# In-chunk product with v as the stationary operand, on two column halves, and the loop re-ordered around it

## The chip, the cores and the metric

The kernel runs on one NeuronCore of a Trainium2 chip. The metric is the time of one execution in microseconds (us): 279.82 us, the median of three runs from 279.08 to 280.14 us. The engines are named as in the profile: PE is TensorE (matmuls; PEld its weight loads), DVE is VectorE, ACT is ScalarE, POOL is GpSimd, and SP is the engine that issues most transfers. SBUF is the working memory of 128 partitions. PSUM is the memory that PE writes to, in eight banks of 128 x 512 float32.

## The reference

The program computes three layers, one after another, on 2 batches of 768 tokens with 8 heads of 40 (width 320). The first is a gated recurrence. Its core, cut:

```
for t in range(S):
    m_new = np.maximum(f_gate[:, :, t] + m, i_gate[:, :, t])
    f_stab, i_stab = np.exp(f_gate[:, :, t] + m - m_new), np.exp(i_gate[:, :, t] - m_new)
    C = f_stab * C + i_stab * einsum('bhd,bhe->bhde', vt, kt)
    n = f_stab * n + i_stab * kt
    y[t] = sigmoid(o_gate[t]) * (C @ qt) / max(abs(n . qt), 1.0)
```

The second layer multiplies by `w_in` (320 x 1024) with a relu, splits the result into halves u and v, normalises v over its 512 columns, mixes v over the tokens with `w_spatial` (768 x 768), multiplies by u, and multiplies by `w_out` (512 x 320). The third multiplies by a second `w_in`, applies a convolution of three taps with a gate, and multiplies by a second `w_out`.

## The kernel before

The recurrence is computed in chunks of L = 128 tokens: NS = 12 chunks (6 for each batch), and a Python loop over the steps n = 1 to 11 writes the instructions of every engine out by hand. Nothing is scheduled by a program: each engine works through its own list in order and waits on semaphores. A step holds one chunk of the recurrence, and beside it pieces of the second layer for earlier chunks. In step n PE does, in this order:

- `scores(n)` (L506): k times q for 8 heads, 8 matmuls with 40 rows each, for even and odd heads in two row halves of the array.
- `transpose_x(n - 1)` (L542): three transposes of x, the finished output of the recurrence for chunk n-1.
- `from_state(n)` (L514): q times the state that chunk n-1 left. It is left out at n = 6, the first chunk of the second batch.
- `in_chunk(n, 0)` (L536): scores times decay is the stationary operand (128 x 128), and `v_aug` (v with two more columns for the denominator, 42 columns for a head) the moving one: 4 matmuls for 4 heads. The result `intra` is 128 tokens by 8 x 42.
- `hidden_v(n - 1)` (L559): 8 matmuls of x with the v half of `w_in`, 512 columns wide.
- `in_chunk(n, 1)`, and `to_state(n + 1)` (L525): k times v for the next state.
- `hidden_u` (L578): 16 matmuls of x of two chunks with the u half.

A float32 matmul appears as two rows in the profile, a transpose and a float32r matmul as one.

DVE multiplies the scores by the decay (`weigh`, L983), splits x (`xt_low`, L1084 and L1086), weighs what comes from the state (`weigh_inter`, L1058), makes the new state (`new_state`, L1051), takes mean and variance of an earlier chunk's hidden v (`moments`, L1091), writes the low part of its normalised v (`vn_low(n - 3)`, L1104) and of a piece of `w_spatial` (`spatial_low`, L1179, from step 6 on), and then combines: numerator (L1065 or L1067), denominator (L1069), reciprocal (L1071), their product (L1073), and x by the output gate (L1079).

ACT splits x as well (`xt_high`, L758 and L759), normalises v of chunk n-3 into z (L774) and copies z to float32r (`vn_high`, L781), applies the relu of u (L768), computes the decay matrices of the next chunk with 8 exponentials of 128 x 128 (`exp_log`, L751, two groups of four), and the relu of v (`v_relus`, L786). In steps 5 to 10 it also rounds a piece of `w_spatial` (`spatial_high`, L791). POOL masks the logarithms, weighs k, decays the state and takes the power for the deviation (L387).

After the loop come 16 `spatial` products (L592) with the rest of layer two between them, and then layer three (L634 and L649).

Of the kernel before, what the change touches and what calls it, by code (L numbers as in the profile page):

```python
# [9 lines left out]
L = 128  # L10
NC = S // L
NS = B * NC
G = 2
# [42 lines left out]
def build_program(nc, qk, k, v, ig, fg, og, w_in, w_sp, b_sp, w_out, w_in2, conv, w_out2, neg_m, out):  # L56
    sems = {}

    def sem(name):
        if name not in sems:  # L60
# [28 lines left out]
             for i, at in enumerate((vn_at, vnlo_at))]  # L89
    o_gate = lambda n: og_b0[:, n, :] if n < NC else og_b1[(n - NC) // 3][:, n % 3, :]  # L90
# [102 lines left out]
    intra = banks[3][:, 0:H * DV].rearrange("p (h d) -> p h d", h=H)  # L193
# [6 lines left out]
    p_cols = banks[4].rearrange("p (i r) -> p i r", i=4)  # L200
    p_mix, p_x = banks[0:2], banks[2:8]
# [6 lines left out]
    by_head = lambda i, n: cols[:, i, n * H:(n + 1) * H].rearrange("p (g j) -> p j g", g=G)  # L208
    pairs = lambda t: t.rearrange("p (j g) d -> p j g d", g=G)
    spatial_step = lambda c: 5 + c  # L210
# [6 lines left out]
    heads = lambda t: t.rearrange("p (h d) -> p h d", h=H)  # L217
# [24 lines left out]
    def sync_program(sp):  # L242
# [22 lines left out]
        def load_v(n):  # L265
            if n >= RING:
                sp.wait_ge(sem("intra_ready"), 2 * (n - RING + 1))
            sp.dma_start(v_aug[n % RING][:, :, :].rearrange("p h d -> p (h d)"), v[n, :, :]
                         ).then_inc(sem(f"ld_v{n % RING}"), 16)
# [17 lines left out]
        load_qk(0)  # L287
        load_in(v_half, "v")
        load_v(0)
# [17 lines left out]
        for n in range(1, NS):  # L307
            if gives_state(n) and ki(n) + KRING < B * (NC - 1):
                load_k(state_chunk(ki(n) + KRING))
            if n + RING < NS:  # L310
                load_qk(n + RING)
                load_log(n + RING)
                load_v(n + RING)
# [25 lines left out]
    def gpsimd_program(pool):  # L339
# [62 lines left out]
        narrow_low(0, v_half)  # L402
        pool.wait_ge(sem("cols_ready"), 4)
        weigh_k(0)
        mask_first(1, 0)
        mask_first(1, 1)
        mask_log(2)
        weigh_k(1)
        decay_state(1)
        weigh_k(2)  # L410
        decay_state(2)
        for n in range(2, NS):
            if n == 2:
                pool.wait_ge(sem("x_ready"), 2)
            if n + 1 < NS:
                mask_log(n + 1)
            if n == 2:
                narrow_low(1, u_half)
            if gives_state(n + 1):
                weigh_k(n + 1)  # L420
                if has_state(n + 1):
                    decay_state(n + 1)
            if n > spatial_step(0):
                spatial_low(n - 1 - spatial_step(0))
            if n > 1:
                deviation(n - 2)
# [23 lines left out]
    def tensor_program(pe):  # L450
        def keep_warm(times):
            for _ in range(times):
                pe.matmul(p_warm[:, 0:2 * L], xt_hi[0][:, 0, 0:128], xt_hi[0][:, 0, :], start=True, stop=True)
# [213 lines left out]
        for n in range(1, NS):  # L667
            scores(n)
            if n == 2:
                from_state(n)  # L670
            transpose_x(n - 1)
            if has_state(n) and n != 2:
                from_state(n)
            in_chunk(n, 0)
            hidden_v(n - 1)
            if n == 1:
                to_state(n)
            in_chunk(n, 1)
            if gives_state(n + 1):
                to_state(n + 1)  # L680
            if n > 1:
                hidden_u(group(n - 2), n % 2)
# [31 lines left out]
    def scalar_program(act):  # L714
# [39 lines left out]
        def xt_high(n):  # L754
# [4 lines left out]
            act.activation(xt5[p][0:K5, cs], p_t[0:K5, 2 * L:3 * L], ACT.Copy).then_inc(sem("xt_hi_ready"), 1)  # L759

# [99 lines left out]
        def narrow_copy(half, cs):  # L860
# [8 lines left out]
        act.activation(win5_lo[LO:128, :].rearrange("p (x t) -> p x t", x=8),  # L869
                       ident[LO:128, :].unsqueeze(1).to_broadcast([LO, 8, 128]), ACT.Copy, scale=0.0).then_inc(sem("win_ready"), 1)  # L870
        narrow_high("v", v_half)
        win_high("v", v_half)
        pad_log(0)
        exp_log(1, 0)
        narrow_copy("v", v_half)
        for n in range(1, NS):
            if n == LATE + 1:
                xt_high(n - 1)
            exp_log(n, 1)
            if n == 1:  # L880
                xt_high(0)
            if n == 2:
                win_high("u", u_half)
                narrow_high("u", u_half)
                xt_high(1)
                narrow_copy("u", u_half)
# [3 lines left out]
            if n not in (1, 2, LATE + 1):  # L890
                xt_high(n - 1)
            if n == 2:
                open_gates(1)
            if n > 2:
                normalise(n - 3)
                vn_high(n - 3)
                ut_relu(group(n - 3), (n - 3) % 2)
# [3 lines left out]
            if n + 1 < NS:  # L901
                exp_log(n + 1, 0)
            if n == 1:
                pad_log(1)
            v_relus(n - 1)
        normalise(NS - 3)
        vn_high(NS - 3)
        ut_relu(group(NS - 3), 1)
# [424 lines left out]
```

## Time and profile before

| | |
|---|---|
| median of 3 runs | 279.82 us (279.08 to 280.14) |
| profiled execution, its own time | 278.94 us |
| its span | 277.1 us, so 1.8 us lie around it |
| PE busy | 269.2 us (97%) |
| DVE, ACT, POOL busy | 202.4 (73%), 165.7 (60%), 69.0 us (25%) |
| granted PE clock | 1.00 (2.4 GHz) in every stretch of the loop |
| chain that ended last | PE 83%, DVE 7%, ACT 6%, issue 2%, DMA 1% |

The span has three parts: a start up to step 1 (0 to 15.4 us), the loop (to 108.7 us), and the stages behind it. Busy time of PE counts a matmul to its modelled end, and neighbours overlap; the distance between the starts of two blocks is what a block takes from PE.

### The profile page before, as it was taken

Reading aid. Unit: us, or ns where it says so; the run is one execution under the profiler, and the core shown is the slowest. Engines: PE = TensorE matmul, PEld = TensorE weight load, DVE = VectorE, ACT = ScalarE, POOL = GpSimd, SP = SyncE. Lnnn points to the kernel's source line nnn. Section 1 sums busy time; section 2 is a strip of 40 time slices with the busy share of each in tenths; the row PEclk is TensorE's granted clock in tenths of the full one; section 3 lists DMA queues with packets and bytes.
Section 4 is the critical chain, followed back from the end, with each engine's and each line's share of the span. In section 5 each row is a group of like instructions: output and inputs, shape, how many; then the busy total and the mean of one; then the engine's idle time right before and its main releaser. Section 6 shows DMA issues by size and latency. Waiting matters only on the chain.

```text
span 277.1 us, 5247 instructions
## 1 busy us (share of the span) xinstructions
PE 269.2 (97%) x1959; PEld 257.6 (93%) x1959; DVE 202.4 (73%) x367; ACT 165.7 (60%) x329; POOL 69.0 (25%) x101
## 2 busy tenths in 40 slices
PE   8889999999999999999999999999999999999995
PEld 6777989889999999999999999999999999999995
DVE  5687987787988988655467686456867776876694
ACT  7968877996886664323243212256576567666763
POOL 6484532166454322063000790000000000000000
PEclk9999999999999999999999999999999999999999
DMA  6789975465546000009400000000000000300004
GB/s 176 227 229 285 296 231 196 143 207 160 184 117 228 2 0 2 0 0 269 151 0 2 0 0 2 0 0 0 4 0 2 0 0 2 142 0 4 0 0 146
DMA packets 13258, 23.61 MB, mean 85 GB/s; under 512 B 1968, under 2 KB 7920, under 8 KB 13232
## 3 DMA queue, kind: packets, MB, share of 16 engines
q1 hardware_dynamic: 12832, 22.89, 27.1%
q8 instruction: 16, 0.26, 0.4%
q10 hardware_dynamic: 400, 0.38, 0.4%
q14 instruction: 10, 0.08, 0.1%
HBM read 21.25 MB, written 2.02 MB: 84 GB/s over the span
## 4 chain that ended last, share of the span: by engine, by line
PE 83%; DVE 7%; ACT 6%; issue 2%; DMA 1%; SPq 0%; DVEq 0%; ACTq 0%
PE bank L592 18%; PE bank L649 14%; PE bank L634 14%; PE bank L617 8%; PE bank L578 7%; PE bank L559 7%; PE bank L536 6%; PE bank L506 3%; PE bank L514 2%; PE bank L542 1%; DMA og_b<-og 1%; PE bank L525 1%; DVE win_lo L988 1%; ACT decay L751 1%; DVE decay L983 1%
## 5 line engine op out<-in xcount | busy, mean ns | idle before, releaser
L592 PE MATMUL bank<-wsp_hi,vn_hi 128*128 128x384 f32 x96 | 32.2, 335 | 0.0
L592 PE MATMUL bank<-wsp_lo,vn_hi 128*128 128x384 f32 x96 | 32.1, 334 | 0.0
L592 PE MATMUL bank<-wsp_hi,vn_lo 128*128 128x384 f32 x96 | 32.1, 334 | 0.0
L796 ACT ACTIVATE gt_hi<-gated_t 128x384 fp32r<-128x384 f32 x16 | 8.4, 524 | 37.1 <-DVE gated_t L1117 37.1
L649 PE MATMUL bank<-wo_hi,hg_hi 128*128 128x320 f32 x96 | 29.8, 311 | 0.3 <-DVE hg_lo L1167 0.3
L649 PE MATMUL bank<-wo_lo,hg_hi 128*128 128x320 f32 x96 | 29.6, 308 | 0.0
L649 PE MATMUL bank<-wo_hi,hg_lo 128*128 128x320 f32 x96 | 29.6, 308 | 0.0
L1150 DVE SCALAR_TENSOR_TENSOR tap<-h,conv_w,tap 128x768 f32<-128x768 f32 (+1 forms) x17 | 16.5, 970 | 17.5 <-ACT tap L828 17.5
L751 ACT ACTIVATE decay<-log_in,cols 128x128 f32<-128x128 f32 x80 | 25.5, 391 | 4.1 <-PE bank L536 4.0
L536 PEld LDWEIGHTS bank<-v_aug,decay 128*128 128x128 f32 x192 | 24.0, 191 | 2.6 <-DVE decay L983 1.3
L834 ACT ACTIVATE gate<-convd 128x768 f32<-128x768 f32 (+1 forms) x17 | 13.8, 809 | 19.3 <-DVE convd L1154 19.3
L536 PE MATMUL bank<-v_aug,decay 128*128 128x42 f32 x192 | 24.3, 278 | 1.0 <-DVE decay L983 0.6
L387 POOL TENSOR_TENSOR rstd<-var_eps,minus_half 128x1 f32<-128x1 f32 x12 | 9.7, 805 | 50.8 <-DVE var_eps L1095 50.8
L634 PE MATMUL bank<-x_hi,win_hi 128*128 128x384 f32 x64 | 21.4, 335 | 0.0
L634 PE MATMUL bank<-x_lo,win_hi 128*128 128x384 f32 x64 | 21.4, 335 | 0.0
L634 PE MATMUL bank<-x_hi,win_lo 128*128 128x384 f32 x64 | 21.4, 335 | 0.0
L983 DVE TENSOR_TENSOR decay<-bank,decay 128x512 f32<-128x512 f32 x24 | 16.5, 687 | 4.7 <-PE bank L506 3.2
L817 ACT ACTIVATE h<-bank 128x384 f32<-128x384 f32 x32 | 15.3, 486 | 7.2 <-PE bank L634 7.2
L1113 DVE TENSOR_TENSOR mixed<-bank,bias_sp 128x384 f32<-128x384 f32 x16 | 8.9, 554 | 13.6 <-PE bank L592 13.6
L649 PEld LDWEIGHTS bank<-wo_hi,hg_hi 128*128 128x128 f32 x96 | 18.0, 187 | 0.7 <-issue 0.6
L1161 DVE TENSOR_TENSOR hg<-h,gate 128x768 f32<-128x768 f32 (+1 forms) x17 | 15.5, 910 | 3.7 <-ACT gate L834 3.7
L592 PEld LDWEIGHTS bank<-wsp_lo,vn_hi 128*128 128x128 f32 x96 | 18.0, 188 | 0.0
(171 smaller groups left out, 766.7 us busy)
## 6 DMA issues: line engine op xcount, KB each, us to landing
qk<-qk SPq DMA_DIRECT2D x24, 160.0 KB
log_in<-neg_m SPq DMA_DIRECT2D x10, 256.0 KB, 5.0
wsp_raw<-w_sp SPq DMA_DIRECT2D x6, 384.0 KB, 3.9
win_raw<-w_in SPq DMA_DIRECT2D x4, 512.0 KB, 5.6
v_aug<-v SPq DMA_DIRECT2D x12, 168.0 KB, 4.4
kw<-k SPq DMA_DIRECT2D x10, 160.0 KB, 4.9
out<-y SPq DMA_DIRECT2D x10, 160.0 KB, 1.9
og_b<-og SPq DMA_DIRECT2D x3, 480.0 KB, 9.9
```

The lines of the kernel that those rows point to most:

```text
L536: op = pe.matmul(intra[:, h, :], decay[g][:, j * L:(j + 1) * L], v_aug[n % RING][:, h, :], start=True, stop=True)
L559: op = pe.matmul(p_v[:, :], lhs, rhs, start=(i == 0), stop=(i == len(products) - 1))
L578: op = pe.matmul(p_u[:, d * 2 * L:(d + 1) * 2 * L], lhs, rhs, start=(i == 0), stop=(i == len(products) - 1))
L592: op = pe.matmul(p_mix[m % 2][:, 0:NB], vs[:, b * NC + c, ds_], ws[:, c, ts], start=(i == 0), stop=(i == len(terms) - 1))
L617: op = pe.matmul(p_x[i % 6][:, 0:NB], w, gs, start=(k_ == 0), stop=(k_ == len(products) - 1))
L634: op = pe.matmul(p_h[blk][:, 0:NB], w, xx, start=(i == 0), stop=(i == len(terms) - 1))
L649: op = pe.matmul(p_y[c][:, 0:HD], g[t % 2][:, cs], w[:, t, :], start=(t == 0 and i == 0), stop=(t == KF - 1 and i == 2))
L751: op = act.activation(dst, src, ACT.Exp, bias=cols[:, 2, r:r + 1], scale=1.0 if n else -1.0)
L817: act.activation(h2[t % 2][:, 1 + blk * NB:1 + (blk + 1) * NB], p_h[blk][:, 0:NB], ACT.Relu).then_inc(sem("relu_done"), 1)
L983: dve.tensor_tensor(decay[g][:, :], p_s[g][:, :, :].rearrange("p h t -> p (h t)"), decay[g][:, :], ALU.mult).then_inc(sem("weights_ready"), 1)
L1150: dve.scalar_tensor_tensor(tap01[:, cs], h2[t % 2][:, moved(cs, 1)], cw[:, t, 1:2], tap0[:, cs], ALU.mult, ALU.add).then_inc(sem("tap01_do ...
L1161: dve.tensor_tensor(hg[e % 2][:, cs], h2[e % 2][:, moved(cs, 1)], gate2[e % 2][:, cs], ALU.mult).then_inc(sem("hg_done"), 1)
```

## The change

The product inside a chunk swaps its operands. `v_aug` of one head (128 x 42) is now the stationary operand, and the decayed scores (128 x 128) move. The result is transposed: 42 rows (numerator and denominators) by 128 tokens. Heads with even j go to columns 0 to 41 of the array and PSUM partitions 0 to 41, heads with odd j to columns and partitions 64 to 105. Keys and v of `to_state` had such halves already. ACT copies the result (106 x 512) from PSUM to SBUF (`num_t`), and PE turns it back with four transposes into a bank that from step 2 on is the first bank of the scores. DVE reads it there. Its combining is split into `numerators(n)` (numerator, denominator, reciprocal) and `combine(n)` (the division in its own step, then the gate). `scores(n)` therefore waits for `numer_done`, and `in_chunk` for `numer_moved`.

The lists of all engines are re-ordered, the load of v stands earlier on SP, and v's ring waits for `to_state` too. A memset moves from ACT to DVE. The diff, cut:

```
-    intra = banks[3][:, 0:H * DV].rearrange("p (h d) -> p h d", h=H)
+    intra_t = banks[3].rearrange("p (g x t) -> p g x t", g=G, x=2)
+    turned_bank = lambda n: p_t if n == 0 else p_u if n == 1 else banks[1]
...
         def scores(n):
+            if n > 2:
+                pe.wait_ge(sem("numer_done"), n)
...
         def in_chunk(n, g):
-                wait(pe, sem("numer_done"), n)
+            if n:
+                pe.wait_ge(sem("numer_moved"), n)
             for j in range(HG):
-                h = head(g, j)
-                op = pe.matmul(intra[:, h, :], decay[g][:, j * L:(j + 1) * L], v_aug[n % RING][:, h, :], start=True, stop=True)
+                x_, c = divmod(j, 2)
+                op = pe.matmul(intra_t[c * LO:c * LO + DV, g, x_, :], v_aug[n % RING][:, head(g, j), :],
+                               decay[g][:, j * L:(j + 1) * L], start=True, stop=True)
+        def turn_back(n):
+            pe.wait_ge(sem("numer_moved"), n + 1)
+            for g in range(G):
+                for x_ in range(2):
+                    at = (2 * g + x_) * 128
+                    op = pe.transpose(turned_bank(n)[:, at:at + LO + DV], num_t[:, g, x_, :], ident[0:LO + DV, 0:LO + DV])
+            op.then_inc(sem("numer_turned"), 1)
...
+        for n in range(2, NS):
+            if n > 2:
+                scores(n)
+            transpose_x(n - 1)
+            if has_state(n):
+                from_state(n)
+            elif gives_state(n):
+                to_state(n)
             in_chunk(n, 0)
+            in_chunk(n, 1)
+            if has_state(n) and gives_state(n):
+                to_state(n)
             hidden_v(n - 1)
+            turn_back(n)
+            hidden_u(group(n - 2), n % 2)
...
+        def move_numer(n):
+            act.wait_ge(sem("intra_ready"), 2 * n + 2)
+            wait(act, sem("numer_turned"), n)
+            act.activation(num_t[:, :, :, :], intra_t[0:LO + DV, :, :, :], ACT.Copy).then_inc(sem("numer_moved"), 1)
...
+        for n in range(3, NS):
+            xt_high(n - 1)
+            normalise(n - 3)
+            move_numer(n)
+            if n + 1 < NS:
+                exp_log(n + 1, 0)
+                exp_log(n + 1, 1)
+            v_relus(n - 1)
+            vn_high(n - 3)
...
+        for n in range(2, NS):
             if n > 2:
                 minus_mean(n - 3)
             weigh(n, 0)
+            weigh(n, 1)
             xt_low(n - 1)
             if has_state(n):
                 weigh_inter(n)
+            if gives_state(n):
                 new_state(n)
...
+            moments(n - 2)
             if n > 2:
                 vn_low(n - 3)
             if n > spatial_step(0):
                 spatial_low(n - 1 - spatial_step(0))
+            numerators(n)
+            combine(n)
```

ACT in step 7 of the loop, before (a name with a number behind it is one buffer of a ring; the brackets hold the semaphores waited for):

```order
L758 ACTIVATE xt_hi_90<-bank 128x2x128 [waits ut_raw,xt_raw]
L759 ACTIVATE xt_94<-bank 64x128
L774 ACTIVATE z<-v_relu_95,shift,rstd 128x512 [waits vn_ready,shift_ready]
L781 ACTIVATE vn_hi<-z 128x512 [waits z_ready]
L768 ACTIVATE uT<-bank 128x2x256 [waits ut_raw]
L751 ACTIVATE decay_81<-log_in_100,cols 128x128 [waits intra_ready,log_masked]
L751 ACTIVATE decay_81<-log_in_100,cols 128x128 x3
L786 ACTIVATE v_relu_95<-bank 128x512 [waits z_ready,vh_ready]
L751 ACTIVATE decay_82<-log_in_100,cols 128x128 [waits intra_ready,log_masked]
L751 ACTIVATE decay_82<-log_in_100,cols 128x128 x3
L791 ACTIVATE wsp_hi<-wsp_raw 128x384 [waits ld_wsp3] x2
```

and ACT in the same step now:

```order
L783 ACTIVATE xt_hi_91<-bank 128x2x128 [waits ut_raw,xt_raw]
L784 ACTIVATE xt_95<-bank 64x128
L804 ACTIVATE z<-v_relu_96,shift,rstd 128x512 [waits vn_ready,shift_ready]
L789 ACTIVATE num_t<-bank 106x512 [waits numer_turned,intra_ready]
L776 ACTIVATE decay_82<-log_in_101,cols 128x128 [waits intra_ready,log_masked]
L776 ACTIVATE decay_82<-log_in_101,cols 128x128 x3
L776 ACTIVATE decay_83<-log_in_101,cols 128x128 [waits intra_ready,log_masked]
L776 ACTIVATE decay_83<-log_in_101,cols 128x128 x3
L816 ACTIVATE v_relu_96<-bank 128x512 [waits z_ready,vh_ready]
L811 ACTIVATE vn_hi<-z 128x512 [waits z_ready]
L821 ACTIVATE wsp_hi<-wsp_raw 128x384 [waits ld_wsp2] x2
```

The copy of z to `vn_hi` stood directly behind z. Now the new copy `num_t`, all eight exponentials and the relu of v stand ahead of it.

DVE in the second part of step 7, before:

```order
L1091 BN_STATS stats<-v_relu_95 128x6 [waits v_relu_ready]
L1093 BN_AGGR mv<-stats 128x2 [waits mom1]
L1095 TENSOR_SCALAR var_eps<-mv 128x1 [waits mom2]
L1104 TENSOR_TENSOR vn_lo<-z,vn_hi 128x512 [waits vn_hi_ready]
L1179 TENSOR_TENSOR wsp_lo<-wsp_raw,wsp_hi 128x384 [waits wsp_hi]
L1065 TENSOR_TENSOR numer<-bank,mix 128x336 [waits mix_done,intra_ready]
L1069 SCALAR_TENSOR_TENSOR denom<-numer 128x8 [waits numer_done]
```

and now:

```order
L1128 BN_STATS stats<-v_relu_96 128x6 [waits v_relu_ready]
L1130 BN_AGGR mv<-stats 128x2 [waits mom1]
L1132 TENSOR_SCALAR var_eps<-mv 128x1 [waits mom2]
L1141 TENSOR_TENSOR vn_lo<-z,vn_hi 128x512 [waits vn_hi_ready]
L1216 TENSOR_TENSOR wsp_lo<-wsp_raw,wsp_hi 128x384 [waits wsp_hi]
L1100 TENSOR_TENSOR numer<-bank,mix 128x336 [waits mix_done,numer_turned]
L1104 SCALAR_TENSOR_TENSOR denom<-numer 128x8 [waits numer_done]
```

The order of these rows is the same. The numerator waits for the turned result instead of the product itself.

PE around the product in step 7, before (the first of the eight instructions of `hidden_v` alone):

```order
L514 MATMUL bank<-state_86,qk_73 128x84 [waits mix_done,state_done]
L514 MATMUL bank<-state_86,qk_73 128x84 x3
L536 MATMUL bank<-v_aug_79,decay_81 128x42 [waits numer_done,ld_v1,weights_ready]
L536 MATMUL bank<-v_aug_79,decay_81 128x42 x3
L559 MATMUL bank<-win_hi,xt_hi_90 128x512 [waits v_relu_ready,xt_ready]
```

and now, from `scores` on:

```order
L512 MATMUL bank<-qk_74 128x128 [waits numer_done,weights_ready,ld_qk1]
L512 MATMUL bank<-qk_74 128x128 x7
L558 MATMUL bank<-ident,x 128x128 [waits x_ready]
L558 MATMUL bank<-ident,x 128x128
L558 MATMUL bank<-ident,x 64x128
L520 MATMUL bank<-state_87,qk_74 128x84 [waits mix_done,state_done]
L520 MATMUL bank<-state_87,qk_74 128x84 x3
L543 MATMUL bank<-decay_82,v_aug_80 42x128 [waits numer_moved,ld_v1,weights_ready]
L543 MATMUL bank<-decay_82,v_aug_80 42x128 x3
L543 MATMUL bank<-decay_83,v_aug_80 42x128 [waits numer_moved,weights_ready]
L543 MATMUL bank<-decay_83,v_aug_80 42x128 x3
L531 MATMUL bank<-v_aug_80,kw_76 40x42 [waits ld_v1,state_done,kw_ready]
```

Both halves of the product stand side by side, `to_state` behind them, and `scores` has the wait for `numer_done` that `in_chunk` had.

## Rows read from the trace of the kernel before

**Rows 1.** The chain that ended last, in order of time: start us, us, what

```profile
10.22 1.05 ACT win_lo L869
...
12.91 1.46 DVE win_lo L988
...
48.83 1.28 ACT L751
...
75.59 1.09 PE bank L506 x16
...
78.02 0.86 PE bank L536 x8
78.88 1.92 PE bank L559 x8
80.80 0.82 PE bank L536 x8
...
82.05 2.11 PE bank L578 x16
84.16 1.09 PE bank L506 x16
...
108.74 3.13 PE bank L592 x18
```

**Rows 2.** Step 7: us, busy PE, PEld, DVE, ACT, POOL, clock, DMA share, GB/s

```profile
66.95:75.52 8.57, 8.57 (x84) 7.87 (x83) 7.37 (x18) 6.24 (x16) 4.47 (x5) 1.00 0.55 175
```

**Rows 3.** PE in order of time: start us, us, engine, instruction

```profile
10.17 1.08 PE L483 MATMUL bank<-gate_padded,ident 128*128 128x128 f32 x8
...
33.63 0.55 PE L542 MATMUL bank<-ident,x 128*128 128x128 f32 x3
...
68.05 0.55 PE L542 MATMUL bank<-ident,x 128*128 128x128 f32 x3
68.43 1.02 PE L514 MATMUL bank<-state,qk 104*128 104x84 f32 x8
69.29 1.02 PE L536 MATMUL bank<-v_aug,decay 128*128 128x42 f32 x8
72.98 0.51 PE L525 MATMUL bank<-v_aug,kw 128*40 128x42 f32 x16
```

**Rows 4.** ACT in step 7, in order of time

```profile
69.91 0.63 ACT L781 ACTIVATE vn_hi<-z 128x512 fp32r<-128x512 f32 x1
70.44 0.58 ACT L768 ACTIVATE uT<-bank 128x512 f32<-128x512 f32 x1
70.92 1.27 ACT L751 ACTIVATE decay<-log_in,cols 128x128 f32<-128x128 f32 x4
72.27 0.60 ACT L786 ACTIVATE v_relu<-bank 128x512 f32<-128x512 f32 x1
```

**Rows 5.** DVE in steps 7 and 11, in order of time

```profile
71.98 0.68 DVE L1104 TENSOR_TENSOR vn_lo<-z,vn_hi 128x512 fp32r<-128x512 f32 x1
72.58 0.55 DVE L1179 TENSOR_TENSOR wsp_lo<-wsp_raw,wsp_hi 128x384 fp32r<-128x384 f32 x1
73.09 0.51 DVE L1065 TENSOR_TENSOR numer<-bank,mix 128x336 f32<-128x336 f32 x1
73.63 0.58 DVE L1069 SCALAR_TENSOR_TENSOR denom<-numer 128x8 f32<-128x8 f32 x1
74.25 0.20 DVE L1071 RECIPROCAL rdenom<-denom 128x8 f32<-128x8 f32 x1
74.48 0.77 DVE L1073 TENSOR_TENSOR numer<-numer,rdenom 128x320 f32<-128x320 f32 x1
75.29 0.49 DVE L1079 TENSOR_TENSOR x<-numer,og_b 128x320 f32<-128x320 f32 x1
...
107.33 0.17 DVE L1069 SCALAR_TENSOR_TENSOR denom<-numer 128x8 f32<-128x8 f32 x1
107.78 0.49 DVE L1073 TENSOR_TENSOR numer<-numer,rdenom 128x320 f32<-128x320 f32 x1
```

More of the change, by code:

```diff
@@ L418, in gpsimd_program @@
                 narrow_low(1, u_half)
+            if n > spatial_step(0):
+                spatial_low(n - 1 - spatial_step(0))
             if gives_state(n + 1):
@@ L422, in gpsimd_program @@
                     decay_state(n + 1)
[L423 to L426, printed above, removed]
+            deviation(n - 2)
         deviation(NS - 2)
@@ L451, in keep_warm @@
         def keep_warm(times):
-            for _ in range(times):
-                pe.matmul(p_warm[:, 0:2 * L], xt_hi[0][:, 0, 0:128], xt_hi[0][:, 0, :], start=True, stop=True)
+            for i in range(times):
+                half = slice((i % 2) * 2 * L, (i % 2 + 1) * 2 * L)
+                pe.matmul(p_warm[:, half], xt_hi[0][:, 0, 0:128], xt_hi[0][:, 0, :], start=True, stop=True)
         pe.wait_ge(sem("warm_zero"), 1)
@@ L666, in tensor_program @@
         to_state(0)
-        for n in range(1, NS):
-            scores(n)
-            if n == 2:
+        turn_back(0)
+        scores(1)
+        from_state(1)
+        in_chunk(1, 0)
+        in_chunk(1, 1)
+        to_state(1)
+        transpose_x(0)
+        turn_back(1)
+        scores(2)
+        hidden_v(0)
+        for n in range(2, NS):
[3 more added lines that the diff above has]
+            if has_state(n):
                 from_state(n)
-            transpose_x(n - 1)
-            if has_state(n) and n != 2:
-                from_state(n)
+            elif gives_state(n):
+                to_state(n)
             in_chunk(n, 0)
+            in_chunk(n, 1)
+            if has_state(n) and gives_state(n):
+                to_state(n)
             hidden_v(n - 1)
[L676 to L682, printed above, removed]
+            turn_back(n)
+            hidden_u(group(n - 2), n % 2)
         spatial(0)
@@ L868, in scalar_program @@
         exp_log(0, 1)
-        act.activation(win5_lo[LO:128, :].rearrange("p (x t) -> p x t", x=8),
-                       ident[LO:128, :].unsqueeze(1).to_broadcast([LO, 8, 128]), ACT.Copy, scale=0.0).then_inc(sem("win_ready"), 1)
         narrow_high("v", v_half)
         win_high("v", v_half)
+        exp_log(1, 0)
+        move_numer(0)
+        exp_log(1, 1)
         pad_log(0)
-        exp_log(1, 0)
         narrow_copy("v", v_half)
[L876 to L886, printed above, removed]
+        pad_log(1)
+        move_numer(1)
+        xt_high(0)
+        exp_log(2, 0)
+        exp_log(2, 1)
+        v_relus(0)
+        win_high("u", u_half)
+        xt_high(1)
+        narrow_high("u", u_half)
+        move_numer(2)
+        narrow_copy("u", u_half)
+        exp_log(3, 0)
+        exp_log(3, 1)
+        v_relus(1)
+        open_gates(1)
+        ut_relu(0, 0)
+        for n in range(3, NS):
[7 more added lines that the diff above has]
+            vn_high(n - 3)
             if spatial_step(0) <= n < spatial_step(NC):
@@ L1182, in vector_program @@
         first_low(0, v_half)
-        for n in range(1, NS):
-            combine(n - 1)
-            if n == 1:
-                new_state(0)
+        new_state(0)
+        numerators(0)
+        weigh(1, 0)
+        weigh(1, 1)
+        combine(0)
+        weigh_inter(1)
+        new_state(1)
+        xt_low(0)
+        numerators(1)
+        combine(1)
+        for n in range(2, NS):
             if n > 2:
                 minus_mean(n - 3)
-            if gives_state(n) and n > 2:
-                new_state(n)
             weigh(n, 0)
-            if n == 2:
-                new_state(n)
+            weigh(n, 1)
             xt_low(n - 1)
@@ L1196, in vector_program @@
                 weigh_inter(n)
-            weigh(n, 1)
-            if n == 1:
+            if gives_state(n):
                 new_state(n)
```

59 lines of the change are left out of this document (25 added, 34 removed).

## The prediction

> **What bounds the kernel now.** I read the chain that ended last first: PE carries 83% of it, and from 60 us on the loop is nothing but PE blocks in a row. One step, from `scores` to `scores`, is 84.16 - 75.59 = 8.57 us [rows 1]. The table by stretches says the same of step 7: PE is busy for 8.57 of 8.57 us, DVE for 7.37, ACT for 6.24, and the granted clock is 1.00 [rows 2]. So a step is PE's work, ACT has 2.3 us of air, and DVE 1.2. Then I read each engine in order of time through step 7 [rows 3 to 5], because the change re-orders all lists, and asked of every wait how late its releaser would now be. That, and not the busy shares, decides here.
>
> **What PE saves.** The product takes 0.86 + 0.82 us in a step, 16 instructions of 0.107 us [rows 1]. These have 42 moving columns, and `from_state` takes the same 0.86 us to the next start with 84 [rows 3]: what is paid is the 128-column stationary operand. New: 16 instructions with 42 stationary and 128 moving columns, alternating between two column halves. The trace does not show this form. Its nearest row for moving columns is `scores`: 16 instructions with 128 moving columns on two row halves, 1.09 us with the switch, or 1.16 us to the modelled end [rows 1, 3]. Less its share of switching I take 0.93 us (16 x 0.058, that is 1.16 less a tail of about 0.25, over 16). The upper end is no overlap: 8 instructions of 128 moving on 128 stationary columns take 1.08 us, a little more than the 1.02 us of the old product [rows 3], so 0.11 us each, 1.76 us for 16. The lower end is `to_state`, 16 in column halves in 0.51 us [rows 3], but with a third of the columns. Four transposes come on top: three of x take 0.38 us to the next start [rows 3], so 0.5 us for four. PE then needs 8.57 - 1.68 + 0.93 + 0.5 = 8.32 us, 0.25 less a step. If PE remained the bound, eleven steps would give about 2.8 us.
>
> **The wait that the order creates.** ACT used to write `vn_hi` right behind z, 69.91 us in step 7, when PE was just in the first half of the product [rows 3, 4]. Now the new copy of the result, all eight exponentials and the relu of v stand ahead of it. DVE's list has `vn_low(n - 3)`, which reads `vn_hi`, and `spatial_low` ahead of `numerators(n)`. Behind the numerator hang two things: `scores(n + 1)`, whose bank it frees, and, through denominator, ratio and gate, x for `transpose_x(n)`, which is queued ahead of `from_state` and the product of the next step. The copy on ACT in turn waits for that product. So this is a closed ring through PE, ACT and DVE, and it must be run once a step, however fast PE is.
>
> The Trainium skill bears on it. The page "TensorEngine Tiling (Array Packing)", section "Performance Considerations", says that tiling speeds up TensorE but not the evacuation of PSUM, which may become the bottleneck. It would have the faster product lose what the copy out of PSUM costs. It gives no time here; rows 4 and 5 price it.
>
> **The ring, from transpose to transpose.** PE: hand-over 0.04, transposes to the next start 0.38, `from_state` 0.86, product to its end 1.16 (as `scores`) [rows 3]. Hand-over 0.04. ACT: the copy of 512 columns out of PSUM like that of u, 0.58 us, but the next starts after 0.48; twice four exponentials 2.40 (4 in 1.27, less the overlap of neighbours); relu 0.50; `vn_hi` 0.63 to its end [rows 4]. Hand-over 0.04. DVE: `vn_lo` 0.60, `wsp_lo` 0.51, numerator 0.54 start to start. That is 8.18 us. Denominator 0.21 to 0.62, reciprocal 0.23, ratio 0.53 to 0.81, x 0.49 [rows 5]: the low values are those of step 11, the high ones of step 7, where POOL worked at the same time. Sum 9.64 to 10.33 us. By the other edge, `scores(n + 1)` can end at 8.18 + 0.04 + 1.09 = 9.3 us, so x is later. PE alone would be back at 8.32. The ring wins by 1.3 to 2.0 us, and PE stands idle for them. Before step 6 there is no `spatial_low` on DVE, and the ring is 9.13 to 9.82.
>
> The relu of v does not stretch it: `hidden_v` ends 0.38 + 0.86 + 0.93 + 0.44 + 1.92, with a tail about 4.8 us after the transposes' start, and ACT is through its exponentials only at 5.4. DVE's own work in front (two `weigh`, `xt_low`, `mix`, new state, moments) is done by about 6 us, `vn_hi` comes at 6.5. What ACT has behind `vn_hi` (rounding of `w_spatial`, relu of u) is hidden in the wait of the next step for its transposes.
>
> **The sum.** Eight rings lie between the transposes of steps 3 and 11: three without and five with `spatial_low`, 3 x 9.13 + 5 x 9.64 = 75.6 at the low, 3 x 9.82 + 5 x 10.33 = 81.1 at the high end. After each opening of output gates ACT loads its exponential table, 1.28 us [rows 1]; this now stands in the ring in steps 3 and 5: + 2.56. Step 6 has no `from_state` but `to_state` ahead of the product: - 0.86 + 0.44. From the transposes of step 11 PE is the bound again, its list has no `to_state` and no exponentials follow: 0.38 + 0.86 + 0.93 + 1.92 + 0.5 + 2.11 = 6.7. Together 84.4 to 89.9 us, against 108.74 - 33.63 = 75.1 us before [rows 1, 3]: 9.3 to 14.8 more.
>
> The start, up to the transposes of step 3, I expect to be shorter. Before, the chain went through a memset of 1.05 us on ACT and the split of `w_in` of 1.46 us on DVE, one after another, ahead of the first numerator [rows 1]. The memset goes to DVE, which waits for PE at that time, and the split now runs beside the first copy and turn. Against these 2.5 us stand the copies and turns of chunks 0 and 1, 0.5 us each, of which about half should show. I take 1.6 us less, between 0 and 3. The earlier load of v and its ring's longer wait cost nothing: loads run three chunks ahead. Behind the loop nothing changes: x of chunk 11 is due only after the first `spatial` product of 3.13 us [rows 1].
>
> Sum: middle 12.1 - 1.6 = 10.5 us longer. The profiled execution took 278.94 us, so it gives 289.4; it lies 0.9 below the median of the runs, 279.82 us, and on that scale I predict 290.3 us.
>
> **Rivals.**
> *The halves do not overlap.* Then the product in the ring takes 0.83 us more (1.76 against 0.93), eight times: 6.6 us, 297 us. For it speaks that all 128 rows are in use by both halves, which is not so in `scores`. Against it: 16 instructions of `to_state` in column halves take 0.51 us to their end [rows 3], about 0.03 each, which leaves hardly any room for loads and matmuls of two halves one after another. The Trainium skill, "TensorE: Matmul & The Clock Gate", section on packing small matmuls, states that weight loads overlap running matmuls only where the row group differs; that would give this rival's 297 us. The same page reports a speed-up for column packing, and no row here shows the weight load of 42 beside 128 moving columns.
> *PE remains the bound, faster.* If `vn_hi` were written early enough, each step would be PE's 8.32 us. The point from which it decides: `vn_hi` must be there before 5.3 us after the transposes' start, so that the numerator is ready at PE's return at 7.2; by the rows it comes at 6.5. It would need two fewer groups of exponentials ahead of it. Price: 2.8 us from the steps and 1.6 from the start, 275.4 us. For it: PE is the bound in all of rows 1. Against it: the lists as they stand.
> *The ring is there, but shorter.* If neighbours on ACT and DVE overlap more and POOL never disturbs DVE, 9.0 us a ring with a start that gains 3 us: about 284 us.
> *The ring grows,* with POOL's halves of `spatial_low` now beside DVE's: 0.5 us more in five rings, 293 us. I hold this in the forecast's own range, 286 to 294.5.
>
> **How the numbers follow.** Forecast 0.76 (290.3 us), no overlap 0.10 (297), shorter ring 0.08 (284), PE the bound 0.05 (275.4), the rest, about the same time, 0.01. The range, 285 to 296, leaves out most of the first and last rivals. One measurement of this kernel tells 0.5% (1.4 us) from no change: faster 0.05, same 0.02, slower 0.93.
>
> **What would show it.** In the profile after: PE idle ahead of the transposes of x, released by DVE x, for 1 to 2 us a step, or ahead of `scores` released by the numerator; DVE idle ahead of `vn_lo`, released by ACT `vn_hi`; transposes of x 9.6 to 10.3 us apart in steps 7 to 11; the product's 16 instructions in 1.2 us; the first `spatial` product at 117 to 121 us instead of 108.7, and the stretch behind it as long as before. DVE never waiting for `vn_hi` would prove the ring wrong. The product in 1.9 us would show the halves one after another. An end of the start later than 33.6 us would put my 1.6 us on the wrong side.

## The result, and the profile after

| | before | after |
|---|---|---|
| median of four runs (least, most), us | 279.45 (278.83, 280.14) | 309.13 (307.52, 311.44) |
| profiled execution, its span, us | 278.94, 277.1 | 307.52, 305.8 |
| transposes of x of step 3 start, us | 33.63 | 36.60 |
| first `spatial` product starts, us | 108.74 | 137.11 |
| from there to the end of the span, us | 168.4 | 168.7 |

The ratio is 1.1068, with the interval [1.0986, 1.1149]. A median is over all runs of a kernel, while a ratio and its interval leave out the runs more than 1.5% above the kernel's fastest; without these the medians of e1 and e6 below are 280.92 and 278.32 us. I had predicted 290.3 us in a range of 285 to 296: the sign was right, the size far off. By the profiled executions the span grew by 28.7 us where I had 10.5. The miss of 18.2 lies in two places. The start came 3.0 us later instead of 1.6 earlier (4.6). From the transposes of step 3 to the first `spatial` product it took 100.5 us, where my sum gave 84.4 to 89.9, middle 87.15 (13.4). The rest is 0.3, behind the loop.

The page of the kernel after: busy times, the granted clock in 40 slices, the chain by engine.

```profile
PE 278.8 (91%) x2007; PEld 262.4 (86%) x2007; DVE 207.8 (68%) x368; ACT 169.9 (56%) x340; POOL 66.4 (22%) x101
...
PEclk9998995997776879999999999999999999999999
...
PE 67%; DVE 13%; ACT 12%; issue 5%; DMA 2%; SPq 0%; ACTq 0%; DVEq 0%
```

PE had 83% of the chain before; DVE and ACT now have 25% together. The clock row is the one I had not foreseen: it held 9 in all 40 slices before, and now has eight below that among the first 15. The waits of after (us in total, times, longest):

```profile
DVE vn_lo L1141 <- ACT vn_hi L811: 22.3, 9, 4.4
...
PE bank L512 <- DVE numer L1100: 12.8, 7, 2.4
...
PE bank L558 <- DVE x L1116: 4.7, 7, 2.3
```

These are the three joints of the ring that I predicted, in its order: ACT to DVE, DVE to `scores`, DVE to the transposes. The chain of waits through step 10, which answers to the step of [rows 1]:

```profile
119.76 0.55 PE bank L558 x3
120.30 0.86 PE bank L520 x8
121.16 1.03 PE bank L543 x16
...
122.71 2.45 ACT decay L776 x8
125.16 0.48 ACT v_relu L816
125.64 0.53 ACT vn_hi L811
...
126.80 1.35 DVE wsp_lo L1216
...
128.19 0.52 DVE numer L1100
```

The next transposes start at 130.25, a step of 10.49 us. Compare term by term with my low sum of 9.64. From the transposes to the end of the product PE takes 2.43 us, where I had 2.40; copy, exponentials, relu and numerator stand as written. The new product's 16 instructions take 1.03 us of the chain. One term is off: `wsp_lo` is 1.35 us, where [rows 5] have 0.55. The difference, 0.8, is nearly the whole of 10.49 - 9.64.

Step 10 was the only late step at full clock. Stretches of after: three around step 4, then step 7 beside step 10 (us, busy PE, PEld, DVE, ACT, POOL, clock, DMA share, GB/s); they answer to [rows 2].

```profile
44.00:46.00 2.00, 0.15 (x2) 0.18 (x4) 1.43 (x4) 0.92 (x2) 0.00 (x0) 1.00 0.41 151
46.00:48.00 2.00, 2.00 (x19) 1.74 (x19) 1.59 (x5) 0.00 (x0) 0.00 (x0) 0.59 0.26 83
48.00:50.00 2.00, 2.00 (x12) 1.85 (x12) 1.61 (x4) 1.25 (x3) 0.00 (x0) 0.50 0.00 0
...
82.36:94.84 12.48, 10.71 (x88) 9.51 (x87) 8.08 (x18) 6.63 (x17) 4.51 (x5) 0.77 0.40 118
119.76:130.25 10.49, 8.22 (x88) 7.33 (x88) 7.95 (x20) 6.50 (x17) 1.64 (x2) 1.00 0.00 0
```

PE is busy 0.15 of 2 us, and when it has work again the clock is 0.59, then 0.50: the lower of its two levels, 1.2 GHz. Steps 7 and 10 have the same 88 instructions; at 0.77 they keep PE busy for 10.71 us, at 1.00 for 8.22. What that looks like in order of time, where step 6 ends and step 7 begins (it answers to [rows 3 to 5]):

```profile
77.75 0.69 DVE L1141 TENSOR_TENSOR vn_lo<-z,vn_hi 128x512 fp32r<-128x512 f32 x1 [3.29 <-ACT vn_hi L811]
...
78.21 1.09 POOL L398 TENSOR_TENSOR wsp_lo<-wsp_raw,wsp_hi 128x384 fp32r<-128x384 f32 x1 [2.01 <-ACT wsp_hi L821]
78.35 1.35 DVE L1216 TENSOR_TENSOR wsp_lo<-wsp_raw,wsp_hi 128x384 fp32r<-128x384 f32 x1
...
80.39 2.03 PE L512 MATMUL bank<-qk 40*128 40x128 f32 x16 [2.35 <-DVE numer L1102]
...
82.36 0.90 PE L558 MATMUL bank<-ident,x 128*128 128x128 f32 x3
...
83.05 1.84 PE L520 MATMUL bank<-state,qk 104*128 104x84 f32 x8
...
84.82 1.94 PE L543 MATMUL bank<-decay,v_aug 128*42 128x128 f32 x16
```

Three things stand here at once. DVE waited 3.29 us for `vn_hi`: the ring. DVE's `wsp_lo` and POOL's overlap, and DVE's ends 0.4 us behind POOL's: 1.35 us. PE then stood idle for 2.35 us, and `scores`, transposes, `from_state` and product take 2.03, 0.90, 1.84 and 1.94 us, where [rows 1, 3] have 1.09, 0.55 and 1.02 and step 10 has 1.08 for the product. All four lie in the ring: x was there at 81.74, but at this clock `scores`, which is queued ahead of the transposes, ends only at 82.42, so even the edge that I had as the shorter one (9.3 against 9.64) decides.

The start, in order of time:

```profile
10.91 0.63 ACT L888 ACTIVATE win_hi<-win_raw 64x512 fp32r<-64x512 f32 x1 [0.85 <-DMA win_raw<-w_in]
...
12.53 1.48 DVE L1019 TENSOR_TENSOR win_lo<-win_raw,win_hi 128x1024 fp32r<-128x1024 f32 x1 [0.42 <-ACT win_hi L884]
...
14.74 0.51 DVE L1102 COPY numer<-bank 128x336 f32<-128x336 f32 x1
...
17.00 0.74 POOL L375 TENSOR_TENSOR state_dec<-state,dec 104x336 f32<-104x336 f32 x1
17.09 2.81 DVE L1110 TENSOR_TENSOR numer<-numer,rdenom 128x320 f32<-128x320 f32 x1
17.70 1.14 POOL L387 TENSOR_SCALAR_AFFINE_SELECT log_in<-log_in 128x1024 f32<-128x1024 f32 x1
18.82 0.73 POOL L370 TENSOR_TENSOR kw<-kw,cols 128x320 f32<-128x320 f32 x1
...
20.48 0.55 PE L558 MATMUL bank<-ident,x 128*128 128x128 f32 x3 [2.31 <-DVE x L1116]
...
30.02 2.47 DVE L1019 TENSOR_TENSOR win_lo<-win_raw,win_hi 128x1024 fp32r<-128x1024 f32 x1
```

The ratio takes 0.49 us when nothing is beside it [rows 5]; here 2.81, until POOL's three instructions in a row are over, and PE waits 2.31 us. The split of `w_in`'s second half, 2.47 us, stands ahead of the numerator of chunk 2. It stood there before as well, and took 1.77 us:

```profile
28.14 1.77 DVE L988 TENSOR_TENSOR win_lo<-win_raw,win_hi 128x1024 fp32r<-128x1024 f32 x1
```

The clock fell in the start too, behind PE's wait of 2.31 us. It was 1.00 in this time before. The stretch from there, then the eight instructions of `hidden_v(0)` in the chain:

```profile
20.48:24.00 3.52, 3.52 (x27) 2.98 (x28) 3.11 (x10) 2.91 (x10) 0.75 (x1) 0.78 1.07 253
```

```profile
22.49 3.63 PE bank L575 x8
```

In the run e2 below, which has the same instructions up to step 3, the ratio took as long (2.79 us) and PE waited 2.29 us for x, but the clock stayed at 1.00, `hidden_v(0)` took 2.08 us of the chain, and the transposes of step 3 came at 35.03 us instead of 36.60.

### The profile page after: what moved, and what is told of

Its sections match the earlier page's. It is cut to its first block, busy times and chain, and to the rows that moved or that the text cites. A ratio compares the mean times of both kernels' runs of the same rounds, so it can differ in the third digit from the quotient of the medians.

```text
span 305.8 us, 5384 instructions
## 1 busy us (share of the span) xinstructions
PE 278.8 (91%) x2007; PEld 262.4 (86%) x2007; DVE 207.8 (68%) x368; ACT 169.9 (56%) x340; POOL 66.4 (22%) x101
## 4 chain that ended last, share of the span: by engine, by line
PE 67%; DVE 13%; ACT 12%; issue 5%; DMA 2%; SPq 0%; ACTq 0%; DVEq 0%
PE bank L608 16%; PE bank L665 13%; PE bank L650 13%; PE bank L633 7%; ACT decay L776 5%; PE bank L543 4%; PE bank L575 3%; PE bank L520 3%; PE bank L558 2%; DVE wsp_lo L1216 2%; DVE numer L1110 2%; PE bank L512 2%; DMA win_raw<-w_in 2%; ACT vn_hi L811 2%; DVE numer L1100 1%
## 5 line engine op out<-in xcount | busy, mean ns | idle before, releaser
L512 PE MATMUL bank<-qk 40*128 40x128 f32 (+1 forms) x192 | 15.6, 306 | 15.7 <-DVE numer L1100 12.8
L512 PEld LDWEIGHTS bank<-qk 40*128 40x128 f32 (+1 forms) x192 | 13.3, 205 | 17.6 <-issue 16.5
L776 ACT ACTIVATE decay<-log_in,cols 128x128 f32<-128x128 f32 x80 | 24.6, 394 | 0.1
L1141 DVE TENSOR_TENSOR vn_lo<-z,vn_hi 128x512 fp32r<-128x512 f32 x12 | 8.9, 738 | 22.3 <-ACT vn_hi L811 22.3
L783 ACT ACTIVATE xt_hi<-bank 128x256 fp32r<-128x256 f32 x12 | 4.6, 384 | 28.7 <-PE bank L558 28.7
L608 PEld LDWEIGHTS bank<-wsp_hi,vn_hi 128*128 128x128 f32 x96 | 18.0, 188 | 0.3 <-DVE wsp_lo L1216 0.3
L608 PEld LDWEIGHTS bank<-wsp_hi,vn_lo 128*128 128x128 f32 x96 | 18.0, 188 | 0.0
```

The costliest lines, as they stand in the source:

```text
L512: op = pe.matmul(p_s[g][:, j, :], qk_n[ps, 1, j, :], qk_n[ps, 0, j, :], start=True, stop=True)
L608: op = pe.matmul(p_mix[m % 2][:, 0:NB], vs[:, b * NC + c, ds_], ws[:, c, ts], start=(i == 0), stop=(i == len(terms) - 1))
L776: op = act.activation(dst, src, ACT.Exp, bias=cols[:, 2, r:r + 1], scale=1.0 if n else -1.0)
```

## The experiments

The ratios are to the kernel before. Unless said otherwise an edit is made on the kernel after. "Steps" are the times between the transposes of x of two steps, "the loop" is from those of step 3 to the first `spatial` product: 75.1 us before, 100.5 after.

| run | median us | ratio | clock of the profiled execution |
|---|---|---|---|
| e1_vn_early | 282.45 | 1.0074 [1.0041, 1.0108] | 0.992 |
| e2_numer_first | 286.10 | 1.0243 [1.0211, 1.0275] | 0.994 |
| e3_keep_warm | 298.68 | 1.0681 [1.0621, 1.0742] | 0.994 |
| e4_pool_late | 310.90 | 1.1111 [1.1043, 1.1178] | 0.927 |
| e5_warm_quiet_ring | 292.99 | 1.0500 [1.0440, 1.0561] | 0.988 |
| e6_vn_quiet | 279.87 | 0.9964 [0.9922, 1.0005] | 0.987 |
| e7_vn_start | 277.08 | 0.9914 [0.9879, 0.9950] | 0.998 |
| e8_all | 274.51 | 0.9816 [0.9781, 0.9852] | 1.000 |
| e9_same_half | 283.40 | 1.0142 [1.0088, 1.0196] | 1.000 |
| e10_old_ring | 312.41 | 1.1239 [1.1165, 1.1314] | 0.928 |

### Is it the ring? Cut it at either joint

**e1**, ACT writes `vn_hi` ahead of the copy and the exponentials:

```diff
             normalise(n - 3)
+            vn_high(n - 3)
             move_numer(n)
...
             v_relus(n - 1)
-            vn_high(n - 3)
```

> The changed kernel with one edit: ACT copies z to vn_hi right behind z, ahead of the new copy and the exponentials. Theory 1 (the ring through ACT's list makes PE wait, and the idle time lets the clock fall): the ring opens, each step is PE's 8.3 us, the clock stays at 1.00 from step 4 on, eight steps and the tail take about 73 us instead of 100.5: 280 to 284 us. Rival (the new form of the product with its two copies makes PE slow or lets the clock fall by itself): the clock stays near 0.95 over the span and the time over 295 us.

One line moved takes 26.7 us off the medians, nearly all that the change cost. Steps 3 to 10 are 7.90 to 9.08 us and the loop 74.3. DVE's `vn_lo` waits for nothing now, and the clock is 1.00 in every stretch of 10 us from 40 to 110. What is left over is DVE's tail in steps 7 to 9. In order of time:

```profile
76.42 1.00 POOL L398 TENSOR_TENSOR wsp_lo<-wsp_raw,wsp_hi 128x384 fp32r<-128x384 f32 x1
...
76.75 1.03 DVE L1110 TENSOR_TENSOR numer<-numer,rdenom 128x320 f32<-128x320 f32 x1
...
77.81 0.91 DVE L1116 TENSOR_TENSOR x<-numer,og_b 128x320 f32<-128x320 f32 x1
...
78.77 0.44 PE L558 MATMUL bank<-ident,x 128*128 128x128 f32 x2 [0.89 <-DVE x L1116]
```

Ratio and gate take twice their 0.49 beside POOL, and PE waits 0.89 us for x.

**e2**, the other joint: DVE's numerator goes ahead of the two instructions that wait for ACT:

```diff
             moments(n - 2)
+            numerators(n)
+            combine(n)
             if n > 2:
                 vn_low(n - 3)
             if n > spatial_step(0):
                 spatial_low(n - 1 - spatial_step(0))
-            numerators(n)
-            combine(n)
```

> The changed kernel with one edit on DVE alone: numerators and combine ahead of vn_low and spatial_low, so the ring is cut at its other joint and ACT is left as it is. Theory 1: the numerator is ready at PE's return, 8.3 to 8.6 us a step, 281 to 286 us, though vn_hi is as late as ever. Rival (ACT is simply too full with the copy): DVE waits elsewhere for ACT, over 295 us.

It also ends the ring: 23.0 us less than after, with ACT's order as it was. A cost that sat in ACT's list alone, or in the product, would have stayed. It is slower than e1: in its step 7, which took 10.86 us, the numerator waited 1.19 us for the turned product, the gate ran beside POOL for 1.18 us, and the clock fell to 0.84.

**e10**, the same list made in the kernel *before*, with its old product: `vn_hi` behind both groups of exponentials.

```diff
             if n == LATE + 1:
+                vn_high(n - 4)
                 xt_high(n - 1)
             exp_log(n, 1)
+            if n > 3 and n != LATE + 1:
+                vn_high(n - 4)
...
                 normalise(n - 3)
-                vn_high(n - 3)
...
+        vn_high(NS - 4)
```

> The kernel before, with its own product and its own lists, and one edit: ACT copies z to vn_hi only behind the exponentials of both groups (for steps 0 to 8). Theory 1 (the order of the lists costs the time, not the new product): the same ring arises, by the rows of before 0.38 + 0.86 + 0.86 + 1.92 + 0.82 + 0.25 on PE, 1.2 + 0.63 on ACT, and about 3.1 on DVE: 10.1 us a step instead of 8.57, 291 to 296 us, more where the clock falls in the idle time. Rival (only the new product with its copy has such a ring): 279 to 281 us.

The kernel without any of the change becomes as slow as the one with it, 1.1239. It was expected at 291 to 296 us, more where the clock falls, and lies 16 us above that. In order of time:

```profile
80.71 1.85 PE L536 MATMUL bank<-v_aug,decay 128*128 128x42 f32 x8
...
89.10 0.69 DVE L1107 TENSOR_TENSOR vn_lo<-z,vn_hi 128x512 fp32r<-128x512 f32 x1 [6.04 <-ACT vn_hi L781]
...
92.23 0.55 PE L542 MATMUL bank<-ident,x 128*128 128x128 f32 x3 [1.43 <-DVE x L1082]
```

The step up to there took 13.26 us, at a clock of 0.74; how much of it is the ring and how much the clock was not run apart. So the place of `vn_hi` is enough for the loss, and the form of the product is not needed for it.

### What does the clock cost?

**e3** fills PE's idle time ahead of `scores` with nine matmuls (two instructions each in the trace) of the identity into columns of a bank that nothing reads then:

```diff
+            if n > 3:
+                pe.wait_ge(sem("state_done"), ki(n - 1) + gives_state(n - 1))
+                for _ in range(9):
+                    pe.matmul(banks[0][:, 384:512], ident[:, :], ident[:, :], start=True, stop=True)
```

> The changed kernel with 9 extra float32 matmuls of 128 x 128 into unused columns of a bank, ahead of scores from step 4 on, where PE stands idle for about 2.3 us; the result does not use them. The ring stays. Theory 1: the clock stays at 1.00 and steps 6 to 10 take 10.1 to 10.5 us instead of 12 to 12.8: about 10 us less, 297 to 301 us. Rival (the long steps come from the ring alone, the clock is a reading): 308 to 310 us.

PE does 144 instructions more, and the kernel is 10.45 us faster than after by the medians. The clock is 1.00 in every stretch of 10 us from 40 to 110. One step, by stretch:

```profile
101.88:112.36 10.48, 10.22 (x105) 9.34 (x106) 7.95 (x20) 6.48 (x17) 3.51 (x4) 1.00 0.01 2
```

Steps 6 to 10 are 9.98, 10.48, 10.49, 10.48 and 10.48 us: step 10 of after in every step (step 6, without `from_state`, is shorter as forecast). The loop takes 90.5 us against 100.5, so 10.0 us of the loss in the loop is the clock. In step 4 the extra matmuls themselves stand in the chain, for 2.01 us, so the clock cost is at least this. The busy share no longer tells where the bound is here: PE is busy for 10.22 of 10.48 us, in part with work that means nothing.

### What does POOL cost?

**e4** puts POOL's half of `spatial_low` back behind its scaling of the state, as it was before:

```diff
-            if n > spatial_step(0):
-                spatial_low(n - 1 - spatial_step(0))
             if gives_state(n + 1):
                 weigh_k(n + 1)
                 if has_state(n + 1):
                     decay_state(n + 1)
+            if n > spatial_step(0):
+                spatial_low(n - 1 - spatial_step(0))
```

> The changed kernel with POOL's half of spatial_low put back behind the decay of the state, as it was before the change, so that it no longer runs beside DVE's half. If the two halves together cost DVE 0.84 us in each of five steps (1.35 or 1.39 us against 0.51 us, inside the ring): 4 to 5 us less, 304 to 305 us, perhaps more where the shorter idle time keeps the clock up. Rival (DVE's half is slow because of something else): 309 us.

No gain, where 304 to 305 us were expected; the interval covers the ratio of after. Steps 7 to 10 take 12.70 to 13.13 us, none of them at full clock. The reason in order of time:

```profile
87.37 1.16 POOL L387 TENSOR_SCALAR_AFFINE_SELECT log_in<-log_in 128x1024 f32<-128x1024 f32 x1
87.84 1.94 DVE L1141 TENSOR_TENSOR vn_lo<-z,vn_hi 128x512 fp32r<-128x512 f32 x1 [1.60 <-ACT vn_hi L811]
88.49 0.74 POOL L370 TENSOR_TENSOR kw<-kw,cols 128x320 f32<-128x320 f32 x1
...
89.70 0.55 DVE L1216 TENSOR_TENSOR wsp_lo<-wsp_raw,wsp_hi 128x384 fp32r<-128x384 f32 x1
```

`wsp_lo` is at its 0.55, but now `vn_lo` stands beside the mask and the keys and takes 1.94 instead of 0.69. The collision had moved, not gone.

**e5** takes away all of it: e4's move, a wait that starts POOL's row only after x, and three filling matmuls for the clock:

```diff
+            if n > 2:
+                pool.wait_ge(sem("x_ready"), n)
             if n + 1 < NS:
                 mask_log(n + 1)
```

> The ring as in the changed kernel, with both things that lengthen it taken away: 3 extra matmuls in PE's idle time ahead of scores hold the clock, and POOL waits for x at the head of a step, so that its masks, keys and its half of spatial_low are done before DVE comes to vn_lo. If the ring was right in its terms and only these two were missed, steps 6 to 10 take the predicted 9.64 us (6: 9.2), steps 3 and 4 9.2 to 10.5, and the time is 290 to 293 us. Rival (POOL is not what stretches DVE's operations): steps of 10.5 us and 297 to 299 us.

Here is the bare ring, in order of time:

```profile
93.45 0.69 DVE L1147 TENSOR_TENSOR vn_lo<-z,vn_hi 128x512 fp32r<-128x512 f32 x1 [1.86 <-ACT vn_hi L817]
94.06 0.55 DVE L1222 TENSOR_TENSOR wsp_lo<-wsp_raw,wsp_hi 128x384 fp32r<-128x384 f32 x1
94.64 0.51 DVE L1106 TENSOR_TENSOR numer<-bank,mix 128x336 f32<-128x336 f32 x1
...
95.62 0.49 DVE L1116 TENSOR_TENSOR numer<-numer,rdenom 128x320 f32<-128x320 f32 x1
96.15 0.49 DVE L1122 TENSOR_TENSOR x<-numer,og_b 128x320 f32<-128x320 f32 x1
```

Steps 7 to 10 are 9.68, 9.67, 9.69 and 9.67 us, and my low sum was 9.64; step 6 is 9.18 against 9.22. Against e3 this is 0.8 us a step. Before step 6 three matmuls did not hold the clock (0.79 in 40 to 50 us, 0.87 in 50 to 60), and steps 3 to 5 took 10.63, 11.86 and 10.51 us instead of the expected 9.2 to 10.5, so e5's total is not a clean sum of the parts.

### Can the ring be cut and the rest mended?

**e6** is e1 with e5's two edits on POOL, without filling matmuls; its diff is those two.

> vn_hi early, and POOL waits for x as in the run above. With vn_hi early alone steps 7 and 8 took 9.0 us, since ratio and x on DVE were stretched to 1.03 and 0.91 us beside POOL. Theory (the two engines exclude each other): 8.35 us in all steps, ratio and x 0.49 each, 2 to 3 us less than with vn_hi early alone: 278 to 279 us. Rival (PE's own work): no change, 281 us.

The loop takes 72.0 us, 2.3 less than e1, with steps of about 8.34, PE's own. The medians differ by 2.6 us. In the profiled execution (281.37 us, in the upper part of 276.50 to 282.57) the transposes of step 3 are at 39.06 us: the start took back what the loop gave. One instruction of DVE there, the denominator of chunk 0, lasts 3.78 us, and the clock was 0.68 in 20 to 30 us.

**e7** is e1 with four edits in the start: ACT's two copies of `w_in`'s u half ahead of the relu of v, DVE's split of it ahead of the split of x (`xt_low`), the numerator of chunk 0 taken apart so that its inverse comes behind `weigh(1, 0)` and `weigh(1, 1)`, and POOL's first row behind x:

```diff
         weigh_k(1)
         decay_state(1)
+        pool.wait_ge(sem("x_ready"), 1)
         mask_log(2)
...
-        numerators(0)
+        numer_only(0)
         weigh(1, 0)
         weigh(1, 1)
+        inverse(0)
```

> vn_hi early, and the start changed: POOL waits for x of chunk 0 ahead of the mask of chunk 2, the denominators of chunk 0 stand behind the weights of chunk 1, and w_in's u half is rounded and split ahead of the relu of v and of xt_low(1). Theory (the start is late because a DVE operation of 0.5 us waited 2.8 to 3.6 us for a row of POOL operations, and because the split of 2.47 us stands ahead of the numerator of chunk 2): the transposes of step 3 come at 33 to 34 us instead of 37.0, 3 us less, 278 us. Rival (the start waits for PE and transfers): under 1 us.

Transposes of step 3 at 32.55 us, 4.5 before e1's 37.04; the clock is 1.00 in every stretch of the start, where e1 had 0.86 in 20 to 30 us; the loop is e1's, 74.2. The four were not run apart, so how much each gives is open.

**e8** has all of it: e6 and e7 together.

> vn_hi early, POOL quiet and the start changed together. Theory: both gains add, 275 to 277 us, below the kernel before (279). Rival: what one edit saves, the other had saved already, 278 us.

Faster than both kernels: 0.9816 of before, 34.6 us less than after. The loop takes 72.0 us and begins at 31.86. A step by stretch:

```profile
72.47:80.81 8.34, 8.15 (x87) 7.29 (x87) 7.67 (x20) 6.68 (x17) 4.53 (x5) 1.00 0.67 228
```

This is the gain that I had worked out for PE: 8.32 us a step against 8.57. It is small beside what a late `vn_hi` costs.

### Does the product need its two halves side by side?

**e9** is e1 with the four heads in the order 0, 2, 1, 3, so that two neighbours fall into the same column half:

```diff
-            for j in range(HG):
+            for j in (0, 2, 1, 3):
```

> vn_hi early, and within each group of four heads the order of the product is 0, 2, 1, 3: four instructions on one column half and then four on the other, instead of two and two. If the two halves run at the same time, the 16 instructions take longer than 1.03 us, towards 1.4 to 1.8 us, and the loop of eleven steps 2 to 6 us longer: 283 to 287 us against 281. If only the short weight load makes the new form cheap and the halves never overlap, nothing changes.

The loop takes 74.4 us against 74.3, and a matmul of the product has a mean of 279 ns against 278. Groups by line of e1, then of e9 (busy us, mean ns | idle before):

```profile
L543 PE MATMUL bank<-decay,v_aug 128*42 128x128 f32 x144 | 9.9, 278 | 0.0
```

```profile
L543 PE MATMUL bank<-decay,v_aug 128*42 128x128 f32 x144 | 10.1, 279 | 0.0
```

So alternation of halves is not what makes the product cheap; 0.007 between e9's and e1's ratios has no row in the loop that explains it (the intervals touch only between 1.0088 and 1.0108). e9's shortest run had a granted clock of 1.000 (280.50 us) and its other three 0.986 to 0.988 (283.14 to 283.96); e1's ten runs go from 279.54 us at 1.000 to 286.43 at 0.982, so a handful of runs at other clocks could make such a difference. e9 also ran on another chip than e1. Whether two halves run at the same time is not settled by this.

## Why the prediction was right and wrong

**Right: the mechanism and its place.** The ring through PE, ACT and DVE exists, with the joints that I named; cut at either of two joints it is gone (e1, e2), and put into the old kernel it makes the same loss (e10). Its bare length is 9.67 to 9.69 us (e5) against 9.64. The tail from the transposes of step 11 takes 6.86 us against 6.7, the stretch behind the loop is unchanged, and the bound for PE alone, 8.32, is what e6 and e8 show (8.34).

**Wrong by 10.0 us in the loop, and some 1.6 in the start: the clock, a term that my sum did not have.** I wrote that "PE stands idle" for 1.3 to 2.0 us a step and priced this as waiting only. This is the step that failed: PE's blocks inside the ring were taken from rows at a clock of 1.00, of a PE without gaps, and carried over to one with gaps. After gaps of about 2 us the rows show 0.50, and the four blocks in the ring grow by 0.35 to 0.94 us each. e3 holds the clock up and the 10.0 us are back. Not each gap does it: step 10 of after has PE busy for 8.22 of 10.49 us and a clock of 1.00 all through. What I should have kept was an upper end with PE's blocks at the lower level.

**Wrong by 4.2 us: `spatial_low` on DVE.** This was in my text as the rival "the ring grows", at 0.5 us in each of five rings. The five instructions took 0.84 more than the 0.51 in my sum. The step that failed here is the price. I knew that POOL's half had come beside DVE's, but I took the denominator's and the ratio's stretch in [rows 5] for the size of such a collision. It is set by how much of POOL's work is still to come when DVE's begins. The page "SBUF — State Buffer" of the Trainium skill, section "Who interferes with whom", says that a DVE instruction with two inputs in SBUF contends with a GpSimd one that reads SBUF, and calls their shared ports an exclusive lock. The trace agrees for `wsp_lo` (0.55 alone, 1.35 beside POOL's 1.09). It also shows the wait lasting over several: the ratio of chunk 0 waited through what was left of three POOL instructions, 2.81 us.

With these two my sum closes. The loop is 90.5 us in e3; less 4.2 it is 86.3, inside the 84.4 to 89.9 of the forecast, and 86.3 + 4.2 + 10.0 = 100.5. The two are 14.2 us where the loop missed by 13.4, since 86.3 lies 0.85 below my middle.

**Wrong by 4.6 us: the start.** I gave it 1.6 us for the memset and the split of `w_in` that were to leave the chain. The memset left ACT, but then the transfer of `w_in` came last: the rounding behind it starts at 10.91 us instead of 11.30, 0.4 earlier and not 1.05. The split did not leave: DVE does it, and then the new state, ahead of the first numerator (the chain gives the time as issue), and this numerator starts at 14.74 us, 0.35 later than before. Behind it two `weigh` of chunk 1, 1.25 us, now stand ahead of the ratio of chunk 0, and this ratio fell beside POOL's row: 2.81 us instead of 0.49. So the transposes of x of chunk 0 came at 20.48 us instead of 16.92. The step that failed is "against these 2.5 us stand the copies and turns": of the 2.5 the new order gave back 0.4, and I counted what was added, and not what the new order put ahead of the ratio and beside POOL. About 1.6 of the 4.6 us is the clock again: 3.63 us for `hidden_v(0)` instead of e2's 2.08. e7 brings the start to 32.55 us, 1.1 before the old kernel's; e8's 31.86 is 1.8. My size was that of an order that keeps DVE clear of POOL's row.

**The rivals.** "The halves do not overlap" had 1.76 us for 16 instructions; they take 1.03 in the chain and 1.08 to the modelled end, my 0.93 for their share being 0.1 low. The rule on weight loads and row groups of the Trainium skill ("TensorE: Matmul & The Clock Gate", section on packing small matmuls), which would have given 297 us, does not decide here: the trace shows 0.065 us for an instruction. "PE remains the bound" needed `vn_hi` ahead of the exponentials: that is e1. Where between the two places the ring begins to decide, 5.3 us by my rows, was not run; by the same rows one group of exponentials fewer ahead of `vn_hi` (1.2 us) would reach it from 6.5, and not two as I wrote. But its price of 275.4 us was too good for e1 alone (282.45); only with POOL quiet and the start mended is it reached, by e8 at 274.51.

The split of the miss into 10.0, 4.2 and 4.6 rests on one profiled execution each of after and e3. The four runs of after spread over 3.9 us and those of e3 over 3.0. The start alone varies: in the six profiles with the same instructions up to step 3 (after, e1, e2, e3, e4 and, with four heads in another order, e9) its transposes come at 35.03 to 39.16 us. So each of the sizes may be off by 1 to 2 us; that all three are there, and that the clock in the loop is the largest, is not in doubt.

## What to carry to other kernels

When a re-ordered list creates a wait in the loop, follow it round: if it closes into a ring over several engines, its length is the step, and moving one instruction of the ring ahead of what it does not need can be worth more than the change itself. Durations read from a kernel whose PE never stops need not hold once it waits; for a forecast in which PE waits, put its blocks at the lower clock level into the upper end. Before pricing a DVE instruction with two SBUF inputs at its undisturbed time, look at what POOL's list has beside it, and for how long.

## What the runs showed of the hardware that I had not expected

- More work on PE made the kernel faster: 144 instructions (72 float32 matmuls) without use, 309.13 to 298.68 us, through the granted clock.
- DVE instructions with all inputs in SBUF were held by a whole row of POOL's back-to-back instructions (ratio 2.81 us in after, denominator 3.78 us in e6; alone 0.49 and 0.17), and by a mask, which has a single input, too: in e1 a denominator of 0.51 us beside one. The numerator, which has one of its two inputs in PSUM, stayed at 0.51 us at 92.78 in after, with POOL's scaling of the keys beside it from 92.30 to 93.35.
- An instruction with 42 stationary and 128 moving columns costs about 0.065 us (1.03 over 16) at full clock, close to the 128 moving columns of `scores` (1.09 over 16), and the two orders of column halves that were run gave it the same mean, 278 and 279 ns.
